# Expert slots of a mixture layer: TensorE's 128x128 transposes replaced by VectorE's 32x32 block transposes and DMA exchanges between partition quarters

## What is computed

```
logits = x @ w_gate                      # 512 -> 8 experts
for each token: e = argmax of logits, or the previous token's e
    h = max(x @ w1[e], 0)                # 512 -> 1024   "first products"
    out = softmax(logits)[e] * (h @ w2[e])   # 1024 -> 512   "second products"
```

## Time and profile before

| | us |
|---|---|
| median of 3 runs | 746.84 (746.83 to 748.22) |
| span of the profiled execution | 746.1 |
| experts' stage, from the first first product to the last y copy | 220.8 to 530.7 |
| TensorE busy in the span | 735.4 |
| VectorE, ScalarE, GpSimd busy in the span | 432.8, 322.1, 329.1 |

### The profile page before, as it was taken

The page is one execution under the profiler, slowest core; times in us unless marked ns, Lnnn a source line. Parts: engine busy times, 40 slices in busy tenths (PEclk is TensorE's granted clock), DMA queues, the critical chain, the costliest instruction groups (busy, mean ns, idle before and its releaser), DMA issues.

```text
span 746.1 us, 15123 instructions
## 1 busy us (share of the span) xinstructions
PE 735.4 (99%) x4971; PEld 626.7 (84%) x4971; DVE 432.8 (58%) x1042; ACT 322.1 (43%) x635; POOL 329.1 (44%) x442
## 2 busy tenths in 40 slices
PE   8999999999989999999999999999999999999998
PEld 6788887887887888888888888888899889889986
DVE  5777878878776544444444545454399455636510
ACT  5777878878430112212121311100397345535620
POOL 7759788887325469444444854400521100000000
PEclk9999999999999999999999999999999999999999
DMA  7888879984064666333334543200421110000011
GB/s 161 206 211 224 230 204 217 239 223 124 17 200 142 232 193 249 144 127 142 127 141 127 171 160 119 89 29 29 139 62 33 43 36 15 29 29 14 29 43 56
DMA packets 99848, 93.39 MB, mean 125 GB/s; under 512 B 62124, under 2 KB 71620, under 8 KB 99780
## 3 DMA queue, kind: packets, MB, share of 16 engines
q1 hardware_dynamic: 79252, 46.51, 22.9%
q10 hardware_dynamic: 17056, 34.69, 13.6%
q0 software_dynamic: 3472, 11.28, 5.3%
HBM read 76.13 MB, written 16.33 MB: 124 GB/s over the span
## 4 chain that ended last, share of the span: by engine, by line
PE 70%; DVE 1%; DMA 0%; issue 0%; ACT 0%; POOLq 0%; DVEq 0%; ACTq 0%
PE row_bank L1306 19%; PE wide_bank L1289 18%; PE wide_bank L1551 14%; PE row_bank L1589 13%; PE wide_bank L1327 3%; PE bank L1255 1%; PE bank L1520 1%; DMA x_slots<-x_rows,token_of 0%; PE bank L1540 0%; PE wide_bank L28 0%; PE row_bank L1540 0%; PE bank L1017 0%; DVE y_sb L1411 0%; DVE xs_tr L1376 0%; DVE xs_tr L1374 0%
## 5 line engine op out<-in xcount | busy, mean ns | idle before, releaser
L912 POOL TENSOR_TENSOR ring<-raw_w,ring 128x2048 fp32r<-128x2048 f32 x28 | 128.6, 4614 | 87.7 <-ACT ring L902 87.7
L1289 PE MATMUL wide_bank<-ring,xs_tr 128*128 x600 | 143.3, 394 | 0.7 <-DVE xs_tr L1368 0.4
L1306 PE MATMUL row_bank<-ring,h_tr 128*128 x600 | 143.5, 394 | 0.0
L902 ACT ACTIVATE ring<-raw_w 128x2048 fp32r<-128x2048 f32 x30 | 55.8, 1908 | 200.3 <-DMA raw_w<-in_moe_w_dram 169.6
L1306 PEld LDWEIGHTS row_bank<-ring,h_tr 128*128 128x128 f32 x600 | 110.8, 188 | 22.7
L1289 PEld LDWEIGHTS wide_bank<-ring,xs_tr 128*128 128x128 f32 x600 | 110.7, 188 | 22.9 <-issue 1.1
L1551 PE MATMUL wide_bank<-x_tr,ring 128*128 128x288 f32 x768 | 107.7, 297 | 0.0
L1551 PEld LDWEIGHTS wide_bank<-x_tr,ring 128*128 128x128 f32 x768 | 103.2, 188 | 0.9
L1589 PE MATMUL row_bank<-ring,g_tr 128*128 128x512 f32 x432 | 100.1, 389 | 0.0
L1589 PEld LDWEIGHTS row_bank<-ring,g_tr 128*128 128x128 f32 x432 | 80.5, 188 | 16.1
L692 ACT ACTIVATE prob<-score,row_min 128x128 f32<-128x128 f32 (+2 forms) x144 | 83.4, 580 | 17.9 <-DVE row_min L555 14.6
(11 more groups left out here) (236 smaller groups left out, 1009.5 us busy)
## 6 DMA issues: line engine op xcount, KB each, us to landing
raw_w<-in_moe_w_dram ACTq DMA_DIRECT2D x12, 2048.0 KB, 8.8
ncum_row<-cum_rows SPq DMA_DIRECT2D x15, 512.0 KB, 5.6
y_sorted<-y_sb SPq DMA_DIRECT2D x26, 256.0 KB
raw_w<-in_moe_w_dram SPq DMA_DIRECT2D x12, 512.0 KB, 3.9
ncum_tail<-cum_rows SPq DMA_DIRECT2D x32, 144.0 KB, 4.4
out_dram<-out_sb ACTq DMA_DIRECT2D x18, 256.0 KB, 2.0
v_nat<-in_v_dram SPq DMA_DIRECT2D x32, 128.0 KB, 3.0
q_nat<-in_q_dram SPq DMA_DIRECT2D x30, 128.0 KB, 4.0
```

Of the source, the lines that this page charges most:

```text
L902: nc.scalar.activation(high, whole, ACT.Copy).then_inc(high_ready, 1)
L912: nc.gpsimd.tensor_tensor(low, whole, high.bitcast(F32), ALU.subtract).then_inc(low_ready, 1)
L1289: last = nc.tensor.matmul(h_bank[:, half, :], xs_tr[:, a, kb, :], ring[:, bass.ds(n, 1), b, at:at + FH].rearrange("p a c -> p (a c)"), sta ...
L1306: last = nc.tensor.matmul(y_bank[:, :], h_tr[:, a, kb, :], ring[:, bass.ds(n, 1), 2 + b, kb * D:(kb + 1) * D].rearrange("p a c -> p (a c)" ...
```

## The change

Slots 0 and 1 and the hidden rows of slot 24 are still turned by TensorE (the change renumbers which input row each block holds, with `every_fourth` and another arrangement of the w1 loads, so that both ways give the same sums). For the tokens of slots 2 to 24 and the hidden rows of slots 2 to 23 the transposes are split into two parts. VectorE's `transpose` turns each block of 32x32 inside its group of 32 partitions, and DMAs move blocks between the four groups ("quarters") of partitions:

- **Tokens**: SyncE writes `x_slots[:, s]` to a DRAM buffer `x_turn[s]` (`x_write`, 256 KB) and reads it back, exchanged, with four DMAs, one for each quarter (`x_read`). VectorE then turns the blocks into `late` (`move_x_blocks`) and splits them into high and low parts from SBUF.
- **Hidden rows**: VectorE turns the blocks of `h_bank` straight into `h_sb` (`h_blocks`, two instructions). SyncE moves them to `h_swapped`, which lies over slots 0 to 3 of `x_slots`, with 16 DMAs of 32 partitions x 1 KB (`h_exchange`). `move_h_blocks` applies the maximum with 0 and splits into `h_tr`, four instructions that read SBUF with a step of 8 elements.
- **Order**: `output(s - 2)` follows `hidden(s)`, where it was `output(s - 1)`. The y sums alternate between two banks.
- **w1 loads** read whole rows (16 KB for a partition in one piece, where it was 4 pieces of 4 KB).

The core of the diff, with the lines after the change in their new form:

```diff
+        def x_write(s):
+            n, i = s % 2, (s - BY_PE) // 2
+            sp.wait_ge(slot_loaded[n], 16 * (s // 2 + 1))
+            above(sp, x_out[n], 16 * i)
+            sp.dma_start(x_turn[s], x_slots[:, s, :]).then_inc(x_out[n], 16)
+
+        def x_read(s):
+            n, i = s % 2, (s - BY_PE) // 2
+            sp.wait_ge(x_out[n], 16 * (i + 1))
+            above(sp, x_back[n], 16 * QUARTERS * i)
+            for g in range(QUARTERS):
+                sp.dma_start(x_slots[g * Q:(g + 1) * Q, s, :].rearrange("p (i c) -> p i c", i=QUARTERS),
+                             x_turn[s][:, g * P:(g + 1) * P].rearrange("(i r) c -> r i c", r=Q)).then_inc(x_back[n], 16)
+
+        def h_exchange(s):
+            n, i = s % 2, s - BY_PE
+            sp.wait_ge(h_ready, 2 * s + 2)
+            above(sp, h_back, 16 * QUARTERS * QUARTERS * i)
+            if i >= 2:
+                sp.wait_ge(ht_ready, 2 * s - 2)
+            for g in range(QUARTERS):
+                for i in range(QUARTERS):
+                    sp.dma_start(h_swapped[n][g * Q:(g + 1) * Q, i * F // QUARTERS:(i + 1) * F // QUARTERS],
+                                 h_sb[i * Q:(i + 1) * Q, g * F // QUARTERS:(g + 1) * F // QUARTERS]).then_inc(h_back, 16)
...
+        def x_swap(begin, end):
+            for s in range(begin, end):
+                if s < SLOTS:
+                    x_write(s)
+                if BY_PE <= s - 1:
+                    x_read(s - 1)
+
+        x_swap(BY_PE, 9)
+        y_store(0)
+        x_swap(9, 12)
+        h_exchange(2)
+        x_swap(12, 15)
+        y_store(1)
+        x_swap(15, 18)
+        h_exchange(3)
+        x_swap(18, 21)
+        h_exchange(4)
+        x_swap(21, SLOTS + 1)
+        for s in range(2, SLOTS - 1):
+            y_store(s)
+            if s + 3 < SLOTS - 1:
+                h_exchange(s + 3)
...
+        hidden(2)
+        output(1)
+        hidden(3)
+        for s in range(4, SLOTS - 1):
+            hidden(s)
+            output(s - 2)
...
+        def h_blocks(s):
+            for half in range(2):
+                dve.wait_ge(h_done, 2 * s + (1 + half))
+                above(dve, h_back, 16 * QUARTERS * QUARTERS * (s - BY_PE))
+                V.transpose(h_sb[:, :].rearrange("p (g r k) -> p g k r", g=QUARTERS, k=KF)[:, :, half * HK:(half + 1) * HK, :],
+                            h_bank[:, half, :].rearrange("p (k g c) -> p g k c", k=HK, g=QUARTERS)).then_inc(h_ready, 1)
...
+        for s in range(2, SLOTS - 1):
+            if s >= 4:
+                move_h_blocks(s - 2)
+            if s != 4 and s != 2:
+                move_y(s - 3 if s > 4 else 1)
+            h_blocks(s)
+            move_x_blocks(s + 1)
```

More of the change, by code:

```diff
@@ L1179, in mixture @@
     y_sb = sb("y_sb", [P, D], where=region)
-    h_bank, ht_bank, x_bank, y_bank = wide_bank[0], wide_bank[1], bank[0], row_bank[0]
+    h_bank, ht_bank, x_bank, y_banks = wide_bank[0], wide_bank[1], bank[0], (row_bank[0], bank[0])
+    BY_PE = 2
+    h_swapped = [x_slots[:, 2 * n:2 * n + 2, :].rearrange("p s d -> p (s d)") for n in range(2)]
+    x_out, x_back = [sem(f"x_out{n}") for n in range(2)], [sem(f"x_back{n}") for n in range(2)]
+    x_blocks, h_back, y_begun = sem("x_blocks"), sem("h_back"), sem("y_begun")
     HK = KF // 2
+    Q = 32
+    QUARTERS = P // Q
     FH = F // 2
@@ L1217, in next_weights @@
             act.wait_ge(h_done, 2 * slots)
[L1218 removed]
+            load_weights(act, n, 0, first, e is not E)
             high_parts(act, n, i, 0)
@@ L1339, in tensor_experts @@
         turn_h(0)
-        for s in range(1, SLOTS - 1):
-            hidden(s, loaded=n if s == 1 else None)
-            turn_x(s + 1, (s + 1) % 2, (s + 1) // 2)
-            output(s - 1)
-            turn_h(s)
+        hidden(1, loaded=n)
+        output(0)
+        turn_h(1)
+        hidden(2)
[4 more added lines that the diff above has]
+            output(s - 2)
         s = SLOTS - 1
         hidden(s, (0,))
+        output(s - 2)
         output(s - 1)
```

88 lines of the change are left out of this document (62 added, 26 removed).

## The result

The changed kernel takes 890.38 us (median of 4 runs, 884.7 to 895.7) against 746.84: a ratio of 1.192, 95% interval 1.187 to 1.197. Forecast were 792 and at most 832. The direction and the parts that would cost time were right, their size was not: +143.5 instead of +45.

A forecast was written before the change was run, and what follows sets the result against it. TensorE, 99% busy, bounded the kernel at 12.27 us a slot. Start 36.0, 17 slots +7.3 and the end about 2 made +45 on 746.1: 791, or 792 with 0.7 between span and median; range 750 to 832.

The forecast's parts named there:

- The circle through h_sb: Slot loop: one h_sb makes transposes, 16 issues, landing and semaphores one round of 12.0 us, bounds 8.9 and 14.9.
- Issues: SyncE's 16 DMA issues for each hidden-row exchange: 0.53 us from start to start, 8.0 us, bounds 5.7 and 9.6.
- Transposes: VectorE's two block transposes of h_bank for each slot: 0.90 us each, 1.8 us together.
- The landing of 2.1: Landing of a hidden-row exchange's last DMA after its issue: 2.1 us, bounds 1.7 and 3.0.
- GpSimd holding VectorE: Slot loop: pairs of GpSimd low parts hold VectorE's SBUF instructions; 12 us over some 12 pairs, 0.7 a slot.
- The start: Up to hidden(7): exchanges stand behind token steps on SyncE; 30.4 us late, 36.0 with one more output behind it.
- The clock: Early slots: gaps of 8 to 17 us may lower TensorE's clock; nothing added for it.
- VectorE's own load: VectorE's instructions in one slot: together 8.3 of 12.0 us, 3.7 free.
- The rules of the Trainium skill: Starting a DMA is usually small beside the DMA; steps up to 4 fp32 are free, giving token transposes 0.69 us.
- The rivals: Whole kernel: cheap exchange 742 (0.12); cheap issues with holds 750 to 766 (0.14); long round (0.10); evening out (0.04).
- The long round: Rival: issues 0.64, landing 2.5 to 3.0, all steps paid; round 14.4, +82 us, 829; chance 0.10.

The follow-up runs named there:

- e17: e2 with two buffers for h_sb from slot 5 on and the same 16 issues, against e2; 793.3 us.
- e2: Changed kernel with GpSimd's low parts of experts 2 to 7, w_in and w_out shrunk to 8 columns, ScalarE copying raw weights instead (values not the reference's); 854.2 us.
- e3: Changed kernel with e2's edit plus hidden rows sent by 4 larger transfers that exchange nothing (values not the reference's); 762.6 us.
- e4: Changed kernel with only SyncE's order altered: exchanges 2, 3 and 4 behind the token steps up to slots 8, 10 and 12; 872.7 us.
- e12: Changed kernel with tokens turned by TensorE as before, so no token issues on SyncE; hidden rows still by 16 transfers; 855.8 us.

## Why the prediction was wrong in size

- **The circle through h_sb.** Right as a mechanism (e17 against e2), too small as a term: 12.0 us forecast, 14.5 in quiet slots and 14.7 in e2. Issues were 0.63 to 0.71 us from start to start, 0.66 in the mean, not 0.53 (10.0 to 11.3 for 16); I had taken the nearest row of another pattern, and my upper bound of 0.64 lay under the mean. Transposes were 1.13 each, not 0.90 (bound 1.10). The landing of 2.1 was right in the middle (1.9), but not beside a load of weights, where it was up to 7.3 with a bound of 3.0. This term gives 17 x (14.5 - 12.27) = 38 us where I had next to none, because 12.0 lay just under the 12.27 of before.
- **GpSimd holding VectorE.** Right in kind (I read it from one instruction of 1.52 us), wrong by the largest factor: 0.7 us a slot forecast, bounds up to 3 for a pair. Of the 76.8 us lost in the slots the 38 above leave 39, 2.3 a slot, for the holds together with TensorE's waits for a low part itself (23.0 us, which I had at nothing here) and some 8 us of late landings; e2, without low parts, has 36 less in these slots. The holds' own share is not measured. I had priced a pair as one hold of 6.9 us, much of it in free time. The trace has VectorE's instructions each held in turn, and the time "free" was on the path: behind `move_h_blocks` stand `h_blocks` and the tokens for the next product, so each hold moves the next exchange. Two terms that I added had to be taken as one chain: e3 shows 37 us that neither removal shows alone.
- **The start.** 59 us instead of 30. Exchange 2 went out at 261.0, not 250.8, because SyncE, which waits in order, stood for landings of token steps: 15.7 us where I had 1.4, less 5.3 that the issues took less than I had. The delay grew from 10 us there to 13 at `hidden(4)`, 17 at `hidden(5)`, behind an L1474 of 9.76 us and exchange 3's landing of 7.3, and 29 at `hidden(7)`, behind exchange 5's of 6.7 and a hold of 4.87 us. The landings of 11.4, 7.3 and 6.7 us, where I had 2.1, all fell beside a load of weights; no run moves the loads, so that these are the cause is read from the rows and not shown. e4 and e12 each take 32 to 36 us off at this place, as the theory of the order wants.
- **The clock.** I added nothing. Hidden products after a gap took 7.2 to 8.3 us instead of 5.6, in about 12 of the 20 slots from 4 on. No run separates it from the waits. Added up, the stage's products took some 36 us longer than 5.6 each, an estimate of the most that they can have added if all of it lay on the path, and in the round shown none did; it stays open how much of the 143 it is.
- **VectorE's own load** of 8.3 us a slot was right in sum and never the bound: e3 runs at 10.88 us a slot.
- **The rules of the Trainium skill.** On issues ("DMA: Bandwidth & Descriptors", "Issuing engines are not separate DMA queues") the trace disagrees for transfers of 32 KB: 0.6 us to issue, 1.9 to land, and 16 issues are five times the landing. On steps ("SBUF — State Buffer", the note on cachelines) the token transposes with a step of 4 took 1.00 us, not the 0.69 that I had made of a free step; but no run has such a transpose without a step, so that the step is what costs is not shown.
- **The rivals.** Of the four none was near. "The long round" had the round nearly right (14.4) but no holds in it; with the 39 us above it would have been closer, some 868. The range was drawn from terms that each had bounds and were never at their upper bounds together. That was the mistake: a longer round, later weights and more holds feed each other.

## What to carry to other kernels

A buffer that exists once and is filled, sent and landed in each turn makes a circle whose time is the sum of its steps, however idle every engine is; look for it first, and cut it by a copy that frees the buffer early (a write to DRAM did it here, 5 issues for 16) before counting issues. Before work is moved from PSUM reads to SBUF reads on VectorE, count what GpSimd does in back-to-back rows at that time: a VectorE instruction that reads and writes SBUF can be held for a GpSimd instruction, now and then for many in a row (block transposes were not held). And ask of every landing on the path which large load is in flight beside it. Here the best version of the idea (752.3 us) gained 0.9 us in a slot without trouble and lost it again at the start and at changes of expert; the kernel before stays the fastest.
